# Nine attention units instead of eight ahead of the MLP, with scores taken last in each TensorE turn

## The reference

```python
# pooled: means over groups of 4 positions, so 144 positions
q_d, k_d, v_d = (a.reshape(B, H, Sd, 4, D).mean(axis=3) for a in (q, k, v))
out_up = np.repeat(sm_attn(q_d, k_d, v_d), 4, axis=2)
# local: only keys with |i - j| < 4
scores = np.where(mask, scale * np.matmul(q, k.transpose(0, 1, 3, 2)), -1e9)
out_local = softmax(scores) @ v
x = (out_up + out_local)          # as 2304 tokens x 512
h = x @ w_in;  x = (h - np.tanh(h)) @ w_out      # 512 -> 2048 -> 512
h = x @ w2_in; return (h * np.cos(h)) @ w2_out
```

## Time and profile before

| what | value |
|---|---|
| median of 3 runs | 922.24 us (922.23 to 923.3) |
| profiled execution: its own time / its span | 923.0 / 921.1 us |
| mean granted TensorE clock | 0.996 |
| TensorE matmul busy | 907.4 us (99%) |
| VectorE / ScalarE / GpSimd busy | 538.2 / 385.7 / 153.0 us |
| chain that ended last, TensorE's share | 93% |
| mean of one tanh (L621) | 496 ns |

### The profile page before, as it was taken

One profiled execution on the slowest core, in us unless ns is written; L12 is line 12 of the kernel. 1 busy time (PEld: TensorE's weight loads), 2 busy tenths in 40 slices (PEclk: granted clock), 3 DMA queues, 4 the chain that ended last, 5 costly groups with the idle time before them and its releaser, 6 DMA issues.

```text
span 921.1 us, 15864 instructions
## 1 busy us (share of the span) xinstructions
PE 907.4 (99%) x6264; PEld 841.3 (91%) x6264; DVE 538.2 (58%) x1073; ACT 385.7 (42%) x1055; POOL 153.0 (17%) x167
## 2 busy tenths in 40 slices
PE   7999999999999999999999999999999999999998
PEld 5789999999999999999999999999999999999997
DVE  4755553444435445433244797777777777777765
ACT  5744444444334434432222353444443444443433
POOL 6479500100000200000069930000000000000000
PEclk9999999999999999999999999999999999999999
DMA  9693001741002900201043401001001000000000
GB/s 292 217 291 87 1 36 58 163 107 70 1 24 81 205 19 1 92 14 35 35 138 116 149 34 35 35 1 35 35 1 34 35 1 1 35 1 1 35 1 34
DMA packets 24638, 59.57 MB, mean 65 GB/s; under 512 B 2293, under 2 KB 5493, under 8 KB 24565
## 3 DMA queue, kind: packets, MB, share of 16 engines
q1 hardware_dynamic: 22212, 50.01, 16.0%
q0 software_dynamic: 2352, 8.55, 5.3%
HBM read 49.12 MB, written 9.44 MB: 64 GB/s over the span
## 4 chain that ended last, share of the span: by engine, by line
PE 93%; DMA 3%; SPq 1%; POOL 1%; DVE 1%; ACT 1%; issue 1%; DVEq 0%
PE ps L477 43%; PE ps L525 22%; PE ps L506 21%; DMA qk<-qkx_in 2%; PE ps L397 2%; PE ps L448 1%; PE ps L437 1%; PE ps L406 1%; DMA vd<-v_in 1%; PE ps L421 1%; PE ps L415 1%; SPq L276 1%; POOL pair_sums L948 0%; PE ps L392 0%; POOL qkd L950 0%
## 5 line engine op out<-in xcount | busy, mean ns | idle before, releaser
L477 PE MATMUL ps<-xh,wi_hi 128*128 128x384 f32 x768 | 262.7, 342 | 0.0
L477 PE MATMUL ps<-xh,wi_lo 128*128 128x384 f32 x768 | 258.6, 337 | 0.0
L477 PE MATMUL ps<-xl,wi_hi 128*128 128x384 f32 x768 | 257.9, 336 | 0.0
L477 PEld LDWEIGHTS ps<-xh,wi_hi 128*128 128x128 f32 x768 | 144.8, 189 | 6.9 <-issue 1.2
L477 PEld LDWEIGHTS ps<-xl,wi_hi 128*128 128x128 f32 x768 | 144.8, 189 | 4.0
L477 PEld LDWEIGHTS ps<-xh,wi_lo 128*128 128x128 f32 x768 | 144.5, 188 | 0.0
L633 ACT ACTIVATE gh<-rem 128x384 fp32r<-128x384 f32 x96 | 50.5, 526 | 213.3 <-PE ps L525 141.8
L506 PE MATMUL ps<-gh,wo_hi 128*128 128x384 f32 x384 | 132.7, 346 | 0.3 <-DVE x L791 0.2
L506 PE MATMUL ps<-gl,wo_hi 128*128 128x384 f32 x384 | 128.5, 335 | 0.0
L506 PE MATMUL ps<-gh,wo_lo 128*128 128x384 f32 x384 | 128.4, 334 | 0.0
L816 DVE TENSOR_TENSOR fn<-ps,fn 128x384 f32<-128x384 f32 x96 | 53.3, 556 | 126.4 <-ACT fn L621 126.4
(11 more groups left out here) (88 smaller groups left out, 1150.7 us busy)
## 6 DMA issues: line engine op xcount, KB each, us to landing
qk<-qkx_in SPq DMA_DIRECT2D x20, 512.0 KB, 4.8
wi_raw<-w_in_in SPq DMA_DIRECT2D x32, 256.0 KB, 5.4
wo_raw<-w_out_in SPq DMA_DIRECT2D x8, 1024.0 KB, 7.0
qkd<-qkf_in POOLq DMA_DIRECT2D x9, 576.0 KB, 6.6
vb<-vx_in SPq DMA_DIRECT2D x20, 256.0 KB, 3.6
y_between<-stage SPq DMA_DIRECT2D x6, 768.0 KB, 4.2
x<-y_between SPq DMA_DIRECT2D x6, 768.0 KB, 5.1
out<-stage SPq DMA_DIRECT2D x18, 256.0 KB, 2.1
```

The costliest lines, as they stand in the source:

```text
L477: mm = MM(ps[:, h_bank(s), 0:NT], w, xx[:, kc, :], start=(n == 0), stop=(n == last))
```

## The change

`UNITS` of batch 0 becomes five local units and then four pooled ones, and FIRST becomes 9: all nine units run in the prologue, and the tenth (the first local one of batch 1) takes the place that unit FIRST had, with scores within `hidden(0)`; its transposes and mixes now come from `unit_at`, at places 1 and 2. The later units follow at places 3, 8, 13, ... where they had 5, 10, 15, ... In the prologue TensorE takes mixes and transposes first in a turn and the scores last. FILL changes; its sum is unchanged (32 dummy matmuls with those of the last turns). The loads of v for units 3 and 4 are issued ahead of the weights, and the load of q/k for unit FIRST+1 ahead of the last two weight loads.

```diff
-UNITS = [("local", 0, n, 0) for n in range(4)] + [("pooled", 0, i, hs) for hs in range(2) for i in range(2)] + [("local", 0, 4, 0)]
+UNITS = [("local", 0, n, 0) for n in range(NL)] + [("pooled", 0, i, hs) for hs in range(2) for i in range(2)]
...
-FIRST = 8
+FIRST = 9
...
         def unit_at(place, later):
-            u, rest = divmod(place - later, 5)
-            return FIRST + 1 + u if place >= later and rest == 0 and FIRST + 1 + u < NU else None
+            u, rest = divmod(place + 2 - later, 5)
+            return FIRST + u if u >= (later == 0) and rest == 0 and FIRST + u < NU else None
...
-            FILL = {0: 7, 1: 2, 2: 6, 3: 1, 4: 1, 5: 2, 6: 2, 7: 2}
-            for k in range(-1, FIRST + 2):
+            FILL = {0: 7, 1: 2, 2: 6, 3: 1, 4: 1, 5: 1, 6: 2, 7: 2, 8: 2, 9: 2, 10: 3}
+            for k in range(-1, FIRST + 1):
+                if k >= FIRST - 1:
+
+                    pe.wait_ge(gathered, after(6))
+                    keep_warm(FILL[k + 1], banks(5))
+                if 0 <= k - 2:
+                    mixes(k - 2)
+                if 0 <= k - 1:
+                    transposes(k - 1)
                 if k + 1 < FIRST:
                     pe.wait_ge(gathered, after(bank_user(k + 1) + 1))
                     keep_warm(FILL[k + 1], banks(k + 1))
                     if k + 1 == 0:
                         pe.wait_ge(const_ready, 2)
                     scores(k + 1)
-                else:
-
-                    pe.wait_ge(gathered, after(bank_user(FIRST) + 1))
-                    keep_warm({FIRST - 1: 4, FIRST: 2, FIRST + 1: 3}[k], banks(FIRST))
-                if 0 <= k - 2:
-                    mixes(k - 2)
-                if 0 <= k - 1 < FIRST:
-                    transposes(k - 1)
+            keep_warm(FILL[FIRST + 1], banks(5))
+            mixes(FIRST - 1)
...
             for s in range(STEPS):
                 attention(2 * s)
-                if s == 0:
-                    transposes(FIRST)
                 hidden(s + AHEAD)
-                if s == 0:
-                    mixes(FIRST)
                 attention(2 * s + 1)
...
-                if 4 <= k < FIRST:
-                    hi_of_in(0, k - 4)
-                if k == FIRST:
+                if 5 <= k < FIRST:
+                    hi_of_in(0, k - 5)
+                if k == FIRST - 1:
                     split_x(0, 0)
                     split_x(0, 1)
```

More of the change, by code:

```diff
@@ L58 @@
 NU = len(UNITS)
-FIRST = 8
+FIRST = 9
 LOCALS = [u for u in range(NU) if UNITS[u][0] == "local"]
 LBUF = {u: 0 for u in LOCALS}
-LBUF[1], LBUF[2], LBUF[3], LBUF[8] = 1, 2, 3, 4
+LBUF[1], LBUF[2], LBUF[3], LBUF[4] = 1, 2, 3, 4
 LAST_POOLED = [max(u for u in range(NU) if UNITS[u][:2] == ("pooled", b)) for b in range(B)]
@@ L196, in banks @@
         def banks(u):
-            return 2 * (u % 4) if u <= FIRST else 6
+            return 2 * (u % 4) if u < FIRST else 6
         def bank_user(u):
@@ L203, in pr_of @@
         def pr_of(u):
-            return pr_first[u % 3] if u <= FIRST else pr_all
+            return pr_first[u % 3] if u < FIRST else pr_all
         def pt_of(u):
-            return pt_first[u % 3] if u <= FIRST else pr_all
+            return pt_first[u % 3] if u < FIRST else pr_all
         def rows_of(u):
@@ L304, in _ @@
             load_v(0)
-            load_qk(FIRST)
+            load_qk(4)
             load_v(1)
             load_v(2)
+            load_v(3)
+            load_v(4)
             load_wi(0, 0, w_in)
-            load_v(3)
             load_wo(0, 0, w_out)
-            load_v(8)
             load_wi(0, 1, w_in)
             sp.wait_ge(qk_summed, after(2))
-            load_qk(9)
+            load_qk(FIRST)
             load_first_of_four(1)
             load_wo(0, 1, w_out)
-            load_v(9)
+            load_v(FIRST)
             load_wi(0, 2, w_in)
@@ L321, in _ @@
             load_wo(0, 2, w_out)
+            load_qk(FIRST + 1)
             load_wi(0, 3, w_in)
@@ L328, in _ @@
             next_store = 0
+            load_v(FIRST + 1)
             for u in range(FIRST + 1, NU):
-                if 5 * (u - FIRST - 1) >= 2 * FC * (next_store + 1):
+                if 5 * (u - FIRST) - 2 >= 2 * FC * (next_store + 1):
                     store_y(next_store)
@@ L490, in contract @@
                 if m == 0:
-                    order = (2, 3, 0, 1) if s == 0 else range(KC)
-                    for j in order:
-                        if s == 0 and j == 2:
+                    for j in range(KC):
+                        if s == 0 and j == 0:
                             pe.wait_ge(gathered, after(FIRST))
-                        if s == 0 and j == 0:
-                            pe.wait_ge(gathered, after(FIRST + 1))
                         if first and t and j < 2:
@@ L503, in contract @@
                         for n, (w, gg) in enumerate(((hi, g_hi), (lo, g_hi), (hi, g_lo))):
-                            if j == order[0] and n == 2:
+                            if j == 0 and n == 2:
                                 pe.wait_ge(gl_done, after(s + 1))
@@ L586, in exponentials @@
                 sc.wait_ge(maxed, after(u + 1))
-                if u <= FIRST:
+                if u < FIRST:
                     sc.wait_ge(transposed, after(u - 2))
-                elif u > FIRST + 1:
+                elif u > FIRST:
                     sc.wait_ge(mixed, after(u))
@@ L686, in _ @@
                     exponentials(FIRST)
-                if s == 1 - AHEAD:
-                    evacuate(FIRST)
                 attention(2 * s + 1)
@@ L868, in _ @@
                     normalise(k - 1)
+                if k == FIRST:
+                    split_x(0, 0)
+                    split_x(0, 1)
                 if 0 <= k - 2:
@@ L873, in _ @@
                     maximum(k + 1)
-                if k == FIRST:
-                    split_x(0, 0)
-                    split_x(0, 1)
             split_x(0, 2)
@@ L888, in attention @@
                     maximum(now)
-                    if now == FIRST + 1:
-                        gather(FIRST)
                     guard(now)
@@ L937, in _, with sums_of_block @@
             pieces = iter(range(1, 8 * WG * KC))
-            def sums_of_block(u, turn):
+            def sums_of_block(u):
                 i, n = LBUF[u], UNITS[u][2]
@@ L948, in sums_of_block @@
                     TT(two, four[:, :, :, :, 0], four[:, :, :, :, 1], ALU.add).then_inc(pair_summed, 1)
-                    gp.wait_ge(pair_summed, after(2 * turn + hf + 1))
+                    gp.wait_ge(pair_summed, after(2 * u + hf + 1))
                     TT(qkd[:, :, g0:g0 + gn], two[:, :, :, 0], two[:, :, :, 1], ALU.add).then_inc(qk_summed, 1)
@@ L990, in lo_of_out @@
                 TT(wo_lo[n][:, c, :], wo_raw[n][:, c, :], wo_hi[n][:, c, :].bitcast(F32), ALU.subtract).then_inc(wo_split, 1)
-            sums_of_block(0, 0)
-            sums_of_block(1, 1)
+            for u in range(3):
+                sums_of_block(u)
             gp.wait_ge(v_first, 16)
             gp.dma_start(vd[0:QH, :, :].rearrange("p c n -> p (c n)"), v4[0, 2], accum_op=ALU.add).then_inc(v_accumulated, 16)
-            sums_of_block(2, 2)
+            sums_of_block(3)
             gp.wait_ge(v_second, 16)
             gp.dma_start(v_other[0:QH, :], v4[0, 3], accum_op=ALU.add).then_inc(v_accumulated, 16)
-            sums_of_block(3, 3)
-            sums_of_block(FIRST, 4)
+            sums_of_block(4)
             gp.wait_ge(v_accumulated, 32)
@@ L1027, in _ @@
                 lo_of_in(2, c, 13 + c)
-            gp.wait_ge(mixed, after(FIRST + 1))
+            gp.wait_ge(mixed, after(FIRST))
             split_wo(0, 2)
```

## The result

| | before | changed |
|---|---|---|
| median | 922.24 us | 939.58 us (937.8 to 940.33, 4 runs) |
| ratio to before | | 1.018 (95% interval 1.0166 to 1.0194) |
| profiled execution: time / span | 923.0 / 921.1 us | 940.33 / 938.5 us |
| mean granted clock | 0.996 | 0.981 |
| start of hidden(0) | 37.73 us | 57.29 us (forecast 49.5) |

A forecast was written before the change was run, and what follows sets the result against it. TensorE is full from 75 us, so the MLP's start and earlier holes decide. Profiled 923.0 + 11.8 for a later hidden(0) - 2.5 for the opening = 932.3 us, median 931.5; range 927.5 to 936.5.

The forecast's parts named there:

- Late stretch full on both sides, so start of the MLP and holes decide: From 75 us TensorE is busy either way; hidden(0)'s start and TensorE's holes between 37.73 and 75 us set the time.
- The loop is closed once a turn: Prologue: transposes(k-1), scores(k+1), top_score(k+1), normalise(k), transposes(k) form one closed loop, passed once in every turn.
- Length of a turn, 4.2 and 4.1 us: Prologue loop at the full clock: 4.2 us for a local turn, 4.1 for a pooled one, against about 3 before.
- half clock at transposes(0): Prologue: after some 3.5 us idle, TensorE runs transposes(0) and six dummies at half clock, 1.9 us more than at full.
- tail to hidden(0): End of prologue, from the last turn's normalise: gather, splits, evacuations, mixes and transposes in series, 5.2 us, hidden(0) at 49.5.
- rival 1: Clock falls inside the prologue turns too, 1.1 us more each: 934.8 us with three such turns, 940 with all eight; 22%.
- Opening, -2.5 us: Start of the MLP, one unit fewer: hidden(0) to contract(2) takes 24.3 us instead of 26.8; later units wait for nothing.
- The price of gl: MLP opening: gl(0) on VectorE taken at its earlier 2.98 us beside GpSimd's wo_lo; bounds 0.56 and 2.98 us.
- Sum: Whole kernel: profiled 923.0 + 11.8 (prologue) - 2.5 (opening) = 932.3 us, median 931.5; this forecast 50%.
- Rival 3: Prologue turns stay at 3 us and the ninth unit fills a hole: hidden(0) at 36.5, time 918.5 us; 4%.

The follow-up runs named there:

- e1: Changed kernel with TensorE taking the scores first in a prologue turn again, nine units kept; 923.3 us, ratio 1.0008 to the kernel before.
- e2: Kernel before, eight units, with only the turn's order changed: TensorE takes the scores last; 933.25 us, ratio 1.0112.
- e4: Changed kernel with GpSimd's addition into vd held back until unit 2 is normalised; 936.3 us, ratio 1.0152 to the kernel before.
- e5: e1 with the load of v for unit 10 issued ahead of the last two weight loads; 922.07 us, ratio 0.9995 to the kernel before.
- e6: e1 with VectorE taking gl(0) ahead of guard, reciprocal and normalise of unit 9; 922.96 us, ratio 0.9999 to the kernel before.
- e10: e5 and e7 together, plus GpSimd's second pair of wo_lo held back until gl(0) is made; 921.73 us, ratio 0.9996 to the kernel before.
- e7: e1 with dummy matmuls put into three holes of the prologue, 44 dummies instead of 32; 922.43 us, ratio 1.0000 to the kernel before.
- e8: e5, e6 and e7 together; 925.01 us, ratio 1.0020 to the kernel before.
- e3: Changed kernel with dummies moved from behind the transposes to the hole ahead of them, 63 instead of 32; 929.13 us, ratio 1.0073 to the kernel before.

## Why the prediction was right in sign and wrong in size

- **Late stretch full on both sides, so start of the MLP and holes decide:** right.
- **The loop is closed once a turn:** right, shown by the chain after and, with the edit alone, by e1 (16 us back) and e2 (11 us lost).
- **Length of a turn, 4.2 and 4.1 us: the step that failed.** It was worked out at the full clock, and there it is right (4.24 and 4.23 in e4, and 3.6 for unit 4 where I had 3.5), but most turns ran at the half clock, at 5.3 to 5.5 us. Ends of normalise after: 11.93, 18.80, 24.89, 30.37, 33.99, 39.25, 44.68, 50.08 us. Steps beside the forecast:

| to unit | forecast | measured | what the difference is |
|---|---|---|---|
| 1 (from 0) | 7.4 | 6.9 | half clock at transposes(0), as forecast; six dummies took 2.6, not 3.0 |
| 2 | 4.2 | 6.1 | GpSimd's addition into vd (e4) |
| 3 | 4.2 | 5.5 | half clock |
| 4 | 3.5 | 3.6 | full clock |
| 5, 6, 7 | 4.1 each | 5.3, 5.4, 5.4 | half clock |
| tail to hidden(0) | 5.1 | 7.2 | half clock for most of it |

The turns at the half clock and the tail are 7.2 us over the forecast, unit 2 is 1.9 and unit 4 0.1 over it; against that units 0 and 1 came 1.4 earlier. Together these make the 7.8 us by which hidden(0) is later than 49.5.

I had the half clock as rival 1 at 22%, with 1.1 us a turn (measured 1.2 to 1.3), and thought single holes of about 1.4 us too short for it. They were not: in the changed kernel the clock fell at 32.3 us, after holes of 1.31 and 0.43 us, and at 52.7, after 0.18 and 0.96. Nor could the length of a single hole tell: e4's clock stayed at 1.00 through three holes of 1.58 us, one in each turn, and fell only after them, at 30.5. That rival's 940 us for all eight turns lies near the measured 939.6 by luck: four turns and the tail ran at half, not eight turns, and GpSimd's addition and the wait for v, which it does not have, bring 3.2 us. (The upper end of my range was also short by its own sum: five turns at 1.1 us give 937.0, not 936.5.)

- **GpSimd in the prologue:** I took the vector steps from rows with little GpSimd work beside them and did not ask which of its instructions the later turns would meet.
- **Opening, -2.5 us:** 23.9 us from hidden(0) to contract(2) against a forecast of 24.3; the hole before transposes(9) was 0.39 instead of 1.2, since TensorE came later to it (half clock until 59.6), the one for gl 1.45 instead of 2.0, the one of 1.3 before mixes(9) was not there, since contract(0) ran at the half clock up to it, and q/k of unit 10 came in time where I had 0.8. Against before (26.8) that is -2.9. But v of unit 10 had been left behind 2 MB of weights while its use moved two places earlier: 1.60 us, where before there was 0.27 at that place, +1.3. I had said that nothing waits there. The load was issued at 73.4 us and landed 14.0 us later; in e5, issued ahead of the last weights, no load of v in the opening takes over 6.4 us and the wait is gone, so its place in the queue is the cause.
- **The price of gl:** 2.55 us where I took 2.98. e6 and e10 (0.56 and 0.55) show that GpSimd's making of wo_lo holds it. Of the trace of before I said more than it shows: the two overlap and gl takes long, but gl's row begins 0.6 us ahead of wo_lo's, so which of them was first is left open by it.
- **Sum:** 923.0 + 19.6 - 2.9 + 1.3 = 941.0 for a measured 940.3; 0.7 us is not attributed.
- **Rival 3** (turns as short as before give 918.5): e1 has such turns and is at 923.3. It left out the falls of the clock and the late v, and its start of the MLP, 36.5, is too early: in the profiled runs of e7, e8 and e10, with the clock at 1.00 up to the MLP and twelve dummies more, hidden(0) starts at 39.4, 38.5 and 38.3.

## What to carry to other kernels

- When two engines each take their work in a fixed order, write down the loop that the two orders close and count how often it is passed; moving one item behind a wait can turn a loop passed once in two turns into one passed in each, with no instruction added.
- A loop with a hole in every pass has to be priced at TensorE's lower clock too, as soon as a row of the trace shows that clock after a hole. The dummies that helped here stood in the hole (e3), where they keep TensorE busy during the wait, and not behind it, where they lengthen the loop.
- When work moves earlier, list each load that it needs, not only the first.

## What was not expected of the hardware

- Once at half, the clock stayed there from 32.3 to 49.3 us although the holes had shrunk to 0.9 to 1.1 us in turns of 5.4; with dummies in the holes (e3) it never fell in the prologue.
- A VectorE operation on 128x8 numbers took up to 2.71 us instead of 0.17 beside GpSimd's weight work and DMA issues (e8). Not every such meeting costs: the same operation took 0.22 us beside wo_lo in e10, and gl 0.55 beside the DMA issues.
